# Earlier tanh, later read-state copy and other moves in the hand-written order of an attention and two-MoE kernel

## The chip, the cores and the metric

The kernel runs on one NeuronCore of one Trainium2 chip. The metric is the device time of one execution in microseconds (us). TensorE (PE in the profile) multiplies matrices, ScalarE (ACT) computes activation functions, VectorE (DVE) does elementwise work and reductions, GpSimd (POOL) issues the scatters, SyncE (SP) issues most of the loads. The engines run on their own and meet through semaphores; each of them takes its own instructions in the order of the program.

## What is computed

```python
scores = scale * x @ state.T            # per batch (4) and head (8): 512 tokens, 32 states, 64 wide
a = softmax(scores);   xread = a @ state
a2 = softmax(scale * state @ x.T);  sread = a2 @ x
x = concat([xread, sread], axis=2)      # -> 2304 rows of 512
h = x @ w_in                            # 512 -> 2048
g = h * tanh(softplus(h))               # mish
x = g @ w_out                           # 2048 -> 512
# then: normalise, 8 logits per row, argmax expert, out = gate * relu(x @ w1[e]) @ w2[e]
```

All is float32. A product of two float32 matrices is made of three products of a rounded part (hi) and a remainder (lo): hi·hi, lo·hi and hi·lo.

## The kernel before

**Stages.** The first 400 us or so are attention and the first MoE; the rest is a loop over tiles of 128 rows, one after the other, each through its expert. The change touches the first stage alone. There the rows come in four chunks c = 0 to 3 of 512 tokens, one for each batch, and a fifth, z, of 128 rows, the read state `sread` of all batches. The 2048 hidden columns of a chunk are 8 pairs p = 0 to 7 of 256 columns; z has two units of 512 columns, z0 and z1. `SEQ` lists these 34 units in the order in which ACT and DVE work on them: pair v = 8c + p is unit u = v up to v = 26, then come z0 (u = 27), pair 27 (28), z1 (29) and the pairs 28 to 31 (30 to 33).

**Weights.** `xread @ w_in` is computed as attention weights times M, with M = state @ w_in: four blocks M(c, nb) for each chunk. PE makes a block from w_in (L535), ACT writes its hi part (`M_hi`, L957), DVE its lo part (`M_lo`, L1341).

**One unit u of mish** goes through these steps, each of them one instruction over 128 x 1024 numbers:

- PE: `H(v)`, the hidden pair, 12 matmuls into two PSUM banks (L597); HB for z (L622).
- ACT: `mish_t` t, tanh (L1026); `mish_w` w, a square (L1030); `mish_b`, b, two exponentials (L1036, L1038), a seed for a reciprocal; `mish_c` c, a square (L1042); `mish_hi` hi (L1049).
- DVE: `mish_q` q (L1479), after w, which reads the PSUM banks of H for the last time; `mish_e` e (L1484), after b; `mish_r` r (L1489); `mish_g` g (L1496), after c and r; `mish_lo` lo (L1502), after hi.
- PE: `Y(v)`, the product with w_out, 24 matmuls (L641), after lo. A chunk's output gathers in four PSUM banks over its 8 pairs.

**Order.** Each engine's order is written out by hand. PE in iteration v: `H(v + 2)`, side work, `Y(v)`, side work. H(v + 2) waits for q of unit v + 1, since it writes into the banks that q reads. DVE in iteration u: q(u), lo(u - 1), side work, e(u), r(u), side work, g(u), side work. ACT in iteration u before the change: t(u), w(u), hi(u - 1), side work, b(u), side work, c(u), side work, and then t(u + 1).

**Side work**, laid into the iterations by pair number:

- attention of the next chunk: `score` (PE, L506, waits for M_lo of the last block of the present chunk, whose PSUM bank it takes), `scores_out` (ACT, L968), `soft_1` (DVE, L1387 to L1391, after scores_out and behind g of pair 2), `exp_1` (ACT), `soft_3`, `soft_4`, `soft_2` and `soft_5` (DVE), `exp_2` (ACT), `A_hi` and `A_lo` (L986, L1431), `turn_x` (DVE, L1362), `sread` (PE, L551), `sread_scale` (DVE, L1440), `sread_turned` (PE, L562) and `sread_out` (ACT, L994 and L997), the copy of the read state.
- output and routing of the chunk before, called `done`: `y_out` (ACT L1065 and DVE L1520), for which the next chunk's first Y waits, since it writes the same banks; `squares` (ACT, L1078); `route_t` (PE, L684), a transpose of one tile of 128 rows; `turned` (ACT, L1086), its copy out of PSUM; `route_l` (PE, L705), the logits from that copy; `parts_out` (ACT, L1091); `route_s` (PE, L712), after parts_out; `route_k`; `route_a` and `route_b` (DVE, L1528 to L1549 and L1557 to L1574), whose last step is the index by which POOL scatters the chunk.

In chunk 3, PE's iteration v = 28 begins H(30), route_l(2, 3), the first half of Y(28), route_s(2). route_l(2, 3) waits for `turned(2, 3)`, which ACT has in iteration u = 31 behind c(31), before and after the change.

The functions that the change touches, with the lines that the profile names:

Of the kernel before, what the change touches and what calls it, by code (L numbers as in the profile page):

```python
# [41 lines left out]
def build(nc, x, state, w_in, w_out, emb, tau, w1, w2, out):  # L42
# [70 lines left out]
    with ExitStack() as ctx:  # L113
# [383 lines left out]
        def _(pe):  # L497
# [297 lines left out]
            for v in range(B * PC):  # L795
# [28 lines left out]
                if c == 3:  # L824
                    if p == 2:
                        route_t(2, 0)
                    if p == 3:
                        route_l(2, 1)
                        route_t(2, 2)
                    if p == 4:  # L830
                        route_l(2, 3)
                        Y(v, (0,))
                        route_s(2)
                    if p == 5:
                        route_k(2)
                    if p == 6:
                        YB(0)
                    if p == 7:
                        Y(v, (0,))
                        TY(t0)  # L840
                Y(v, (1,) if v == 0 or c in (1, 2) and p == 3 or c == 3 and p in (4, 7) else (0, 1))
                if v < 2:
# [8 lines left out]
                if c == 0:  # L851
                    if p == 3:
                        score(1)
                    if p == 4:
                        sread_turned(0)
# [84 lines left out]
        def _(act):  # L940
# [218 lines left out]
            for u in range(1, PC):  # L1159
                mish_b(u)  # L1160
                if u == 6:
                    o_split(6)
                if u < PC - 1:
                    mish_t(u + 1)
# [3 lines left out]
                if u == PC - 1:  # L1168
                    o_split(7)
                    break  # L1170
                mish_w(u + 1)
                if u == 6:
                    A_hi(1)
# [10 lines left out]
                if u == 4:  # L1184
                    scores_out(1)
                    o_split(5)
                if u == 5:
                    exp_1(1)
                    sread_out(0)
            for u in range(PC, len(SEQ)):  # L1190
                kind, c, p = SEQ[u]
                n = p if kind == "m" else -1
                done = c - 1 if kind == "m" else -1
                mish_t(u)
                if n == (6 if c == 3 else 5):
# [6 lines left out]
                if done >= 0:  # L1202
# [4 lines left out]
                    if n == 5 and c == 3:  # L1207
                        turned(done, 2)
                if kind == "m" and (n in (0, 2) and c == 1 or n == 2 and c > 1):
                    M_hi(c, n + 1)  # L1210
# [6 lines left out]
                if n == 6 and c in (1, 2):  # L1217
                    A_hi(c + 1)
                mish_b(u)
                if (kind, p) == ("z", 1):  # L1220
                    turned(2, 0)
# [6 lines left out]
                if n == 2 and c in (1, 2):  # L1228
                    scores_out(c + 1)
                if done >= 0 and n == 1:  # L1230
                    y_out(done)
                    if c > 1:
                        M_hi(c, 2)
                mish_c(u)
                if c == 1 and n == 0:
                    M_hi(1, 2)
                if done >= 0:
                    if n == 2:
                        squares(done, (0, 1) if c < 3 else range(ST))
                    if n == 3 and c < 3:  # L1240
                        turned(done, 1)
                        squares(done, (2, 3))
                    if n == 4 and c < 3:
                        turned(done, 3)
                    if n == 5:
                        if c == 3:
                            turned(done, 3)
                        else:
                            gate_exp(done)
                    if n == 6 and c == 3:  # L1250
                        gate_exp(done)
                        split_gz(0)
                    if n == 7 and c == 3:
                        split_gz(1)
                if c in (1, 2):
                    if n == 4:
# [78 lines left out]
        def _(dve):  # L1335
# [335 lines left out]
            for u in range(1, PC):  # L1671
                mish_e(u)
                mish_r(u)
                if u == 5:
                    sread_scale(0)
                if u == 6:
# [6 lines left out]
                if u == 6:  # L1683
                    A_lo(1)
                mish_lo(u)
                if u > 1:
                    o_rest(u)
# [16 lines left out]
            for u in range(PC, len(SEQ)):  # L1704
                kind, c, p = SEQ[u]
                n = p if kind == "m" else -1
                done = c - 1 if kind == "m" else -1
                if done >= 0 and n == (7 if c == 3 else 6):
                    route_b(done)
                mish_q(u)  # L1710
                if SEQ[u - 1][0] == "m":
                    mish_lo(u - 1)
                if done >= 0 and n == (6 if c == 3 else 5):
                    route_a(done)
                if n == 7 and c in (1, 2):
                    M_lo(c + 1, 1)
                if kind == "m" and (n in (0, 2) and c == 1 or n == 2 and c > 1):
                    M_lo(c, n + 1)
# [4 lines left out]
                if n == 4 and c in (1, 2):  # L1723
                    soft_2(c + 1)
                mish_e(u)
                mish_r(u)
                if n == 6 and c in (1, 2):
                    M_lo(c + 1, 0)
                if n == 1 and c > 1:
                    M_lo(c, 2)  # L1730
                if done >= 0 and n == 1:
                    y_out(done)
                mish_g(u)
                if n == 0 and c > 1:
                    sread_scale(c)
                if c == 1 and n == 0:
                    M_lo(1, 2)
                if c in (1, 2):
                    if n == 0:
# [11 lines left out]
                if kind == "m" and c < 3:  # L1751
                    if n == 5 and c == 1:
                        sread_scale(1)
                    if n == 5 and c > 0:
                        soft_5(c + 1)
                    if n == 6 and c > 0:
                        A_lo(c + 1)
                if c == 3 and n == 6:
# [170 lines left out]
```

## Time and profile before

| | us |
|---|---|
| median of three runs | 672.82 |
| lowest and highest | 672.47, 672.86 |
| profiled execution | 672.58 |
| its span, first to last instruction | 670.8 |
| PE busy in the span | 644.4 |
| DVE busy | 442.9 |
| ACT busy | 387.4 |

The profiled execution lies between the lowest and the highest run; 1.8 us of it lie around the span. The clock granted to TensorE was 0.996 of full speed over the span. Read the table by engine first: the one that is nearly always busy sets the pace, and what is left to win is the time in which it sits idle and whom it waits for.

### The profile page before, as it was taken

The page shows a single profiled execution, that of the slowest core. Times are in us where ns is not written, and L with a number is a line of the kernel's source. Part 1 is how long each engine was busy: PE and PEld are TensorE (multiplying, and loading weights), DVE is VectorE, ACT ScalarE, POOL GpSimd, SP SyncE. Part 2 cuts the span into 40 slices and gives each one's busy share as a digit, 9 for nine tenths or more (in the row PEclk, how much of TensorE's full clock was granted, in tenths as well). Part 3 has the DMA queues.
Part 4 walks back from the last instruction along what each step waited for, and adds up shares of the span by engine and source line. Part 5 has one row for each costly group of instructions (what it writes and reads, how often), then busy time and mean ns, then how long its engine had stood idle before and what let it go on. Part 6 is the DMA issues. An engine that isn't in the chain of part 4 may idle for free.

```text
span 670.8 us, 12454 instructions
## 1 busy us (share of the span) xinstructions
PE 644.4 (96%) x4174; PEld 496.0 (74%) x4175; DVE 442.9 (66%) x701; ACT 387.4 (58%) x501; POOL 51.0 (8%) x76
## 2 busy tenths in 40 slices
PE   7889999999999999999999999999999999999996
PEld 5666767577776777766678888788888888888884
DVE  6899899978688789775677677654512542272271
ACT  2789678687588685777787473444422531261260
POOL 2000000000200001100000213010000100100101
PEclk8999999999999999999999999999999999999999
DMA  8802546200433000515000632662711441063140
GB/s 256 246 33 95 191 131 199 78 2 2 128 127 95 32 2 33 158 52 192 9 1 1 250 96 97 235 237 88 241 32 38 166 161 47 32 208 136 41 163 6
DMA packets 35352, 72.73 MB, mean 108 GB/s; under 512 B 5700, under 2 KB 5700, under 8 KB 35313
## 3 DMA queue, kind: packets, MB, share of 16 engines
q1 hardware_dynamic: 27728, 56.93, 26.2%
q0 software_dynamic: 3040, 9.13, 3.5%
q10 hardware_dynamic: 4544, 6.14, 3.0%
q8 instruction: 26, 0.43, 0.3%
q14 instruction: 14, 0.11, 0.0%
HBM read 60.92 MB, written 12.16 MB: 109 GB/s over the span
## 4 chain that ended last, share of the span: by engine, by line
PE 65%; DVE 16%; ACT 9%; issue 5%; DMA 3%; ACTq 0%; SPq 0%; POOL 0%; DVEq 0%; POOLq 0%
PE PS L748 16%; PE PS L777 16%; PE PS L641 14%; PE PS L597 5%; DVE ww L1484 3%; PE PS L757 2%; PE PS L506 2%; PE PS L622 2%; ACT ww L1042 2%; DVE qq L1496 2%; ACT rr L1038 2%; DVE qq L1479 2%; PE PS L662 1%; ACT rr L1036 1%; PE PS L535 1%
## 5 line engine op out<-in xcount | busy, mean ns | idle before, releaser
L641 PE MATMUL PS<-WH,gh 128*128 128x512 f32 x256 | 103.9, 406 | 2.1 <-DVE ysb L1520 1.3
L641 PE MATMUL PS<-WH,gl 128*128 128x512 f32 x256 | 101.0, 395 | 0.0
L641 PE MATMUL PS<-WL,gh 128*128 128x512 f32 x256 | 100.9, 394 | 0.0
L1142 ACT ACTIVATE hh<-PS 128x512 fp32r<-128x512 f32 x40 | 21.9, 595 | 91.3 <-PE PS L757 88.2
L1578 DVE TENSOR_TENSOR WL<-raw,WH 128x1024 f32 (+1 forms) x48 | 56.0, 1220 | 19.2 <-ACT WH L1122 18.6
L777 PE MATMUL PS<-WH,hh 128*128 (+1 forms) x160 | 65.3, 408 | 0.0
L777 PE MATMUL PS<-WH,hl 128*128 (+1 forms) x160 | 63.0, 394 | 0.0
L777 PE MATMUL PS<-WL,hh 128*128 (+1 forms) x160 | 62.8, 393 | 0.0
L641 PEld LDWEIGHTS PS<-WH,gh 128*128 128x128 f32 x256 | 48.2, 188 | 19.3 <-issue 8.2
L1597 DVE TENSOR_SCALAR osb<-PS,gid 128x512 f32<-128x512 f32 x21 | 15.7, 749 | 66.8 <-PE PS L777 66.8
L1122 ACT ACTIVATE WH<-raw 128x1024 f32 (+1 forms) x48 | 47.6, 1054 | 20.1 <-issue 7.5
L1042 ACT ACTIVATE ww<-ww,cst 128x1024 f32<-128x1024 f32 (+1 forms) x35 | 39.4, 1126 | 34.1 <-DVE ww L1484 34.1
L641 PEld LDWEIGHTS PS<-WH,gl 128*128 128x128 f32 x256 | 48.2, 188 | 11.3
L1479 DVE SCALAR_TENSOR_TENSOR qq<-ww,PS 128x1024 f32<-128x1024 f32 (+1 forms) x35 | 41.4, 1183 | 22.4 <-ACT ww L1030 22.4
L641 PEld LDWEIGHTS PS<-WL,gh 128*128 128x128 f32 x256 | 48.3, 189 | 10.0
L1134 ACT ACTIVATE hsb<-PS 128x512 f32<-128x512 f32 x42 | 24.3, 593 | 51.8 <-PE PS L748 44.1
L1484 DVE SCALAR_TENSOR_TENSOR ww<-ww,rr 128x1024 f32<-128x1024 f32 (+1 forms) x35 | 41.6, 1188 | 17.8 <-ACT rr L1038 17.7
L748 PE MATMUL PS<-WH,yh 128*128 (+1 forms) x168 | 47.7, 405 | 1.5 <-DVE yl L1583 1.5
L597 PE MATMUL PS<-Ah,WH 128*128 128x512 f32 x124 | 42.7, 425 | 6.1 <-DVE qq L1479 5.1
L1583 DVE TENSOR_TENSOR yl<-PS,yh 128x512 fp32r<-128x512 f32 x21 | 14.4, 688 | 48.2 <-ACT yh L1128 48.2
L1496 DVE SCALAR_TENSOR_TENSOR qq<-ww,qq 128x1024 f32<-128x1024 f32 (+1 forms) x33 | 39.3, 1190 | 10.2 <-ACT ww L1042 10.2
L748 PE MATMUL PS<-WH,yl 128*128 (+1 forms) x168 | 46.0, 395 | 0.0
(275 smaller groups left out, 1245.6 us busy)
## 6 DMA issues: line engine op xcount, KB each, us to landing
raw<-in_w SPq DMA_DIRECT2D x48, 512.0 KB, 3.3
raw<-in_w_in SPq DMA_DIRECT2D x36, 512.0 KB, 4.8
yg<-by_expert ACTq DMA_DIRECT2D x22, 260.0 KB
raw<-in_w_out SPq DMA_DIRECT2D x8, 512.0 KB, 5.0
by_expert<-junk SPq DMA_DIRECT2D x1, 2080.0 KB, 10.1
wr<-in_w_in SPq DMA_DIRECT2D x4, 512.0 KB, 9.1
x_0a<-in_x SPq DMA_DIRECT2D x8, 128.0 KB, 4.3
x_0b<-in_x SPq DMA_DIRECT2D x8, 128.0 KB, 4.8
```

The costliest lines, as they stand in the source:

```text
L597: mm = pe.matmul(PS[:, h_bank(v) + e, :], w[:, (NB * c + p // 2) % NM, o:o + P], a[:, c % 2, g, :], start=(i == 0 and g == 0), stop=(i == ...
L641: mm = pe.matmul(PS[:, 2 + t, :], a[:, v % 2, e, t * P:t * P + P], w[:, 8 + p, e * 512:e * 512 + 512], start=(p == 0 and e == 0 and i == 0 ...
L748: mm = pe.matmul(PS[:, j, :], a[:, k, :], w[:, bass.ds(slot + k, 1), j * 512:j * 512 + 512].rearrange("p o n -> p (o n)"), start=(i == 0 a ...
L777: mm = pe.matmul(PS[:, o_bank(t, end), :], a[:, m, :], w[:, bass.ds(slot + (KT + m // 2), 1), (m % 2) * 512:(m % 2) * 512 + 512].rearrange ...
L1042: a.activation(ww[:, u % 2, es], ww[:, u % 2, es], ACT.Square, bias=cst[:, 0:1]).then_inc(s_rdy, 1)
L1122: a.activation(WH[:, bass.ds(slot + b, 1), :].rearrange("p o n -> p (o n)"), raw[:, b % NSTAGE], ACT.Copy).then_inc(w_hi, 1)
L1134: a.activation(hsb[:, j * 512:j * 512 + 512], PS[:, j, :], ACT.Relu).then_inc(hs_rdy, 1)
L1142: a.activation(hidden(end)[0][:, 4 * j:4 * j + 4, :], PS[:, 3 + j, :].rearrange("p (k m) -> p k m", k=4), ACT.Copy).then_inc(hh_rdy, 1)
L1479: v.scalar_tensor_tensor(out=qq[:, u % 2, es], in0=ww[:, u % 2, es], scalar=4.0, in1=PS[:, bank + es.start:bank + es.stop, :], op0=ALU.sub ...
L1484: v.scalar_tensor_tensor(out=ww[:, u % 2, es], in0=ww[:, u % 2, es], scalar=4.0, in1=rr[:, es], op0=ALU.add, op1=ALU.mult).then_inc(e_rdy, 1)
L1496: v.scalar_tensor_tensor(out=to, in0=ww[:, u % 2, es], scalar=0.75, in1=qq[:, u % 2, es], op0=ALU.add, op1=ALU.mult).then_inc(g_rdy, 1)
L1578: v.tensor_tensor(WL[:, bass.ds(slot + b, 1), :].rearrange("p o n -> p (o n)"), raw[:, b % NSTAGE], WH[:, bass.ds(slot + b, 1), :].rearran ...
```

## The change

No instruction is added or taken away. Moved are:

- ACT, units 8 to 33: tanh of the next unit, t(u + 1), stands ahead of c(u) where the next unit is a pair, at the end of the iteration where it is z. (Up to unit 7 it stood ahead of c already.)
- ACT: `turned(done, 1)` and `turned(done, 3)` of chunks 0 and 1 go ahead of that t and of c; `sread_out(0)` from the end of unit 5 to behind b(6); `exp_1(1)` ahead of hi(5); `y_out(0)` ahead of b(9); `M_hi(1, 3)` from unit 10 to behind b(9).
- DVE: `sread_scale(0)` behind lo(5), `sread_scale(2)` and `(3)` ahead of g; `y_out(0)` ahead of e(9); `M_lo(1, 3)` from unit 10 to behind g(9); `route_b` of chunks 0 and 1 from ahead of q to behind lo; `A_lo(2)` and `A_lo(3)` from behind g to behind that route_b, ahead of e.
- PE: the first half of Y(3) stands behind H(5), `score(1)` between the halves; the first half of Y(26) ahead of route_t(2, 0).

```diff
--- before.py
+++ after.py
@@ -823,6 +823,7 @@
                     M(c + 1, p - 5)
                 if c == 3:
                     if p == 2:
+                        Y(v, (0,))
                         route_t(2, 0)
                     if p == 3:
                         route_l(2, 1)
@@ -838,7 +839,10 @@
                     if p == 7:
                         Y(v, (0,))
                         TY(t0)
-                Y(v, (1,) if v == 0 or c in (1, 2) and p == 3 or c == 3 and p in (4, 7) else (0, 1))
+                if v == 3:
+                    Y(v, (0,))
+                    score(1)
+                Y(v, (1,) if v in (0, 3) or c in (1, 2) and p == 3 or c == 3 and p in (2, 4, 7) else (0, 1))
                 if v < 2:
                     M(0, v + 2)
                 if c in (1, 2):
@@ -849,8 +853,6 @@
                         route_l(c - 1, 2)
                         route_t(c - 1, 3)
                 if c == 0:
-                    if p == 3:
-                        score(1)
                     if p == 4:
                         sread_turned(0)
                 if c < 3:
@@ -1160,6 +1162,7 @@
                 mish_b(u)
                 if u == 6:
                     o_split(6)
+                    sread_out(0)
                 if u < PC - 1:
                     mish_t(u + 1)
                 if u == 6:
@@ -1169,6 +1172,8 @@
                     o_split(7)
                     break
                 mish_w(u + 1)
+                if u == 5:
+                    exp_1(1)
                 if u == 6:
                     A_hi(1)
                 mish_hi(u)
@@ -1184,14 +1189,11 @@
                 if u == 4:
                     scores_out(1)
                     o_split(5)
-                if u == 5:
-                    exp_1(1)
-                    sread_out(0)
+            mish_t(PC)
             for u in range(PC, len(SEQ)):
                 kind, c, p = SEQ[u]
                 n = p if kind == "m" else -1
                 done = c - 1 if kind == "m" else -1
-                mish_t(u)
                 if n == (6 if c == 3 else 5):
                     parts_out(done)
                 mish_w(u)
@@ -1206,7 +1208,7 @@
                         turned(done, 2)
                     if n == 5 and c == 3:
                         turned(done, 2)
-                if kind == "m" and (n in (0, 2) and c == 1 or n == 2 and c > 1):
+                if kind == "m" and (n == 0 and c == 1 or n == 2 and c > 1):
                     M_hi(c, n + 1)
                 if c > 1 and n == 1:
                     sread_out(c)
@@ -1216,7 +1218,13 @@
                     exp_1(c + 1)
                 if n == 6 and c in (1, 2):
                     A_hi(c + 1)
+                if c == 1 and n == 1:
+                    y_out(done)
                 mish_b(u)
+                if c == 1 and n == 1:
+                    M_hi(1, 3)
+                if n in (3, 4) and 0 < c < 3:
+                    turned(done, (1, 3)[n - 3])
                 if (kind, p) == ("z", 1):
                     turned(2, 0)
                 if c == 3 and n == 4:
@@ -1227,10 +1235,11 @@
                     M_hi(c + 1, 0)
                 if n == 2 and c in (1, 2):
                     scores_out(c + 1)
-                if done >= 0 and n == 1:
+                if c > 1 and n == 1:
                     y_out(done)
-                    if c > 1:
-                        M_hi(c, 2)
+                    M_hi(c, 2)
+                if u < LAST and SEQ[u + 1][0] == "m":
+                    mish_t(u + 1)
                 mish_c(u)
                 if c == 1 and n == 0:
                     M_hi(1, 2)
@@ -1238,10 +1247,7 @@
                     if n == 2:
                         squares(done, (0, 1) if c < 3 else range(ST))
                     if n == 3 and c < 3:
-                        turned(done, 1)
                         squares(done, (2, 3))
-                    if n == 4 and c < 3:
-                        turned(done, 3)
                     if n == 5:
                         if c == 3:
                             turned(done, 3)
@@ -1252,6 +1258,8 @@
                         split_gz(0)
                     if n == 7 and c == 3:
                         split_gz(1)
+                if u < LAST and SEQ[u + 1][0] == "z":
+                    mish_t(u + 1)
                 if c in (1, 2):
                     if n == 4:
                         exp_2(c + 1)
@@ -1671,8 +1679,6 @@
             for u in range(1, PC):
                 mish_e(u)
                 mish_r(u)
-                if u == 5:
-                    sread_scale(0)
                 if u == 6:
                     M_lo(1, 0)
                 mish_g(u)
@@ -1683,6 +1689,8 @@
                 if u == 6:
                     A_lo(1)
                 mish_lo(u)
+                if u == 5:
+                    sread_scale(0)
                 if u > 1:
                     o_rest(u)
                 if u == 1:
@@ -1705,16 +1713,19 @@
                 kind, c, p = SEQ[u]
                 n = p if kind == "m" else -1
                 done = c - 1 if kind == "m" else -1
-                if done >= 0 and n == (7 if c == 3 else 6):
+                if c == 3 and n == 7:
                     route_b(done)
                 mish_q(u)
                 if SEQ[u - 1][0] == "m":
                     mish_lo(u - 1)
+                if c in (1, 2) and n == 6:
+                    route_b(done)
+                    A_lo(c + 1)
                 if done >= 0 and n == (6 if c == 3 else 5):
                     route_a(done)
                 if n == 7 and c in (1, 2):
                     M_lo(c + 1, 1)
-                if kind == "m" and (n in (0, 2) and c == 1 or n == 2 and c > 1):
+                if kind == "m" and (n == 0 and c == 1 or n == 2 and c > 1):
                     M_lo(c, n + 1)
                 if c == 1 and n == 0:
                     soft_2(1)
@@ -1722,19 +1733,23 @@
                     soft_5(1)
                 if n == 4 and c in (1, 2):
                     soft_2(c + 1)
+                if c == 1 and n == 1:
+                    y_out(done)
                 mish_e(u)
                 mish_r(u)
                 if n == 6 and c in (1, 2):
                     M_lo(c + 1, 0)
                 if n == 1 and c > 1:
                     M_lo(c, 2)
-                if done >= 0 and n == 1:
+                if c > 1 and n == 1:
                     y_out(done)
-                mish_g(u)
                 if n == 0 and c > 1:
                     sread_scale(c)
+                mish_g(u)
                 if c == 1 and n == 0:
                     M_lo(1, 2)
+                if c == 1 and n == 1:
+                    M_lo(1, 3)
                 if c in (1, 2):
                     if n == 0:
                         turn_x(c + 1, 0)
@@ -1753,8 +1768,6 @@
                         sread_scale(1)
                     if n == 5 and c > 0:
                         soft_5(c + 1)
-                    if n == 6 and c > 0:
-                        A_lo(c + 1)
                 if c == 3 and n == 6:
                     lo_gz(0)
                 if c == 3 and n == 7:
```

## Rows read from the trace of the kernel before

**Rows 1.** Busy time, share of the span and instructions of each engine, from the page.

```profile
PE 644.4 (96%) x4174; PEld 496.0 (74%) x4175; DVE 442.9 (66%) x701; ACT 387.4 (58%) x501; POOL 51.0 (8%) x76
```

**Rows 2.** Timeline of PE, 98 to 335 us: start, duration, instruction [idle before <-releaser].

```profile
99.85 0.71 PE L597 MATMUL PS<-Ah,WH 128*128 128x512 f32 x2 [0.94 <-issue]
...
124.47 0.48 PE L641 MATMUL PS<-WH,gh 128*128 128x512 f32 x1 [1.30 <-DVE ysb L1520]
...
147.40 0.43 PE L705 MATMUL PS<-yTr,enT 128*32 128x128 f32 x8 [1.00 <-ACT yTr L1086]
...
189.03 0.72 PE L597 MATMUL PS<-Ah,WH 128*128 128x512 f32 x2 [0.39 <-DVE qq L1479]
...
237.34 0.43 PE L705 MATMUL PS<-yTr,enT 128*32 128x128 f32 x8 [1.02 <-ACT yTr L1086]
...
264.94 0.74 PE L597 MATMUL PS<-Ah,WH 128*128 128x512 f32 x2 [1.42 <-DVE qq L1479]
...
290.82 0.41 PE L562 MATMUL PS<-ident,shn 128*64 128x128 f32 x2 [0.52 <-DVE shn L1440]
...
333.32 0.63 PE L684 MATMUL PS<-ident,ysb 128*128 128x128 f32 x4 [0.92 <-DVE qq L1479]
```

**Rows 3.** Waits of ACT: engine, line, released by: us in total, times, longest.

```profile
ACT ww L1042 <- DVE ww L1484: 34.1, 27, 2.5
...
ACT ww L1026 <- PE PS L597: 7.9, 7, 1.7
```

**Rows 4.** Timeline of DVE at 98 us: A_lo(1), for which H(8) waits.

```profile
98.53 1.22 DVE L1431 TENSOR_TENSOR Al<-AF,Ah 128x1024 fp32r<-128x1024 f32 x1
```

**Rows 5.** Timeline of PE: end of H(11), route_l(0, 0) behind Y(9), start of H(12).

```profile
136.08 0.62 PE L597 MATMUL PS<-Ah,WL 128*128 128x512 f32 x2
...
142.64 0.43 PE L705 MATMUL PS<-yTr,enT 128*32 128x128 f32 x8
...
143.41 0.71 PE L597 MATMUL PS<-Ah,WH 128*128 128x512 f32 x2
```

**Rows 6.** Timeline of ACT, 134 to 138 us: scores_out(2), c(10), t(11).

```profile
134.01 1.02 ACT L968 ACTIVATE SC<-PS 128x1024 f32<-128x1024 f32 x1 [4.43 <-PE PS L506]
134.94 1.14 ACT L1042 ACTIVATE ww<-ww,cst 128x1024 f32<-128x1024 f32 x1
...
137.35 1.01 ACT L1026 ACTIVATE ww<-PS 128x1024 f32<-128x1024 f32 x1
```

**Rows 7.** Timeline of DVE, 136 to 142 us: g(10), soft_1(2) (first and last of three), q(11).

```profile
136.18 1.22 DVE L1496 SCALAR_TENSOR_TENSOR qq<-ww,qq 128x1024 f32<-128x1024 f32 x1 [2.37 <-ACT ww L1042]
137.32 1.24 DVE L1387 STREAM_TRANSPOSE PT<-SC 128x1024 f32<-128x1024 f32 x1
...
139.92 1.23 DVE L1391 TENSOR_TENSOR PT<-PT,r 128x1024 f32<-128x1024 f32 x1
141.06 1.21 DVE L1479 SCALAR_TENSOR_TENSOR qq<-ww,PS 128x1024 f32<-128x1024 f32 x1
```

**Rows 8.** Timeline of DVE at 219 us: M_lo(2, 3).

```profile
218.88 1.21 DVE L1341 TENSOR_TENSOR WL<-PS,WH 128x1024 fp32r<-128x1024 f32 x1
```

**Rows 9.** Timeline of DVE, 261 to 264 us: route_b(1), first and last of 14.

```profile
261.60 0.15 DVE L1557 TENSOR_REDUCE small<-lg 128x4 f32<-128x32 f32 x1
...
263.59 0.17 DVE L1574 CAST idx<-small 128x4 uint32<-128x4 f32 x1
```

**Rows 10.** Timeline of PE: last matmuls of H(30), then route_l(2, 3).

```profile
353.23 0.61 PE L597 MATMUL PS<-Ah,WL 128*128 128x512 f32 x2
353.77 0.42 PE L705 MATMUL PS<-yTr,enT 128*32 128x128 f32 x8
```

**Rows 11.** Timeline of ACT, 350 to 355 us: c(31), turned(2, 3), t(32).

```profile
350.91 1.15 ACT L1042 ACTIVATE ww<-ww,cst 128x1024 f32<-128x1024 f32 x1 [1.29 <-DVE ww L1484]
351.96 0.58 ACT L1086 ACTIVATE yTr<-PS 128x512 f32<-128x512 f32 x1
353.88 1.03 ACT L1026 ACTIVATE ww<-PS 128x1024 f32<-128x1024 f32 x1 [1.34 <-PE PS L597]
```

## The prediction, made before the changed kernel was run

> **What bounds the kernel now.** I read the page's busy times first. PE is busy for 644.4 of 670.8 us and its clock is 0.996 of full speed, so the time is PE's work plus the places where PE stands still [rows 1]. No instruction is added or dropped, so the change can only move PE's idle time, 26.4 us in the whole span. Next I went through PE's timeline for all of its waits between 98 us, where the change begins to act, and 400 us, where the tile loop takes over. There are eight of more than 0.2 us, 0.94 + 1.30 + 1.00 + 0.39 + 1.02 + 1.42 + 0.52 + 0.92 = 7.5 us [rows 2]. That is all that the change can win. Then the waits of ACT: in front of c it idles 27 times, 34.1 us in all, 1.26 us each, since e on DVE ends that much after b. In front of t it waits for H only 7 times [rows 3]. The change puts t into the first of these holes. What the reader is to see is why the second figure is small: t today comes when H is long done.
>
> **The parts that aim at a wait.** Each is followed by order alone, with the durations of the rows.
>
> - Chunk 0. With score(1) half a Y earlier, scores_out(1) and soft_1(1) start earlier and two holes of DVE close (1.2 and 0.5 us). sread_scale and sread_out leave the way of g(5) and of b(6). A_lo(1) ends at about 98.9 instead of 99.75 us [rows 4], and the wait of H(8), 0.94 us (the page says issue, but it ends 0.1 us after A_lo), nearly goes. PE's order itself costs nothing: score(1) needs an M_lo that is done by then.
> - y_out(0) ahead of e(9) and b(9). Y(8) no longer waits for the copy: 1.30 us gone. M(1, 3)'s split moves with it, so score(2) finds its bank free.
> - turned(., 1) ahead of t: the two waits of 1.00 and 1.02 us at route_l go.
> - route_b behind q and lo: 14 small instructions, from 261.60 to 263.67, 2.1 us [rows 9], leave the way of q(14) and q(22); the waits 0.39 and 1.42 us are theirs.
> - sread_scale(3) ahead of g: 0.52 us. First half of Y(26) ahead of route_t(2, 0), which waits for q of z1: 0.92 us, covered by 2.9 us of matmuls.
>
> Taken alone these would give the full 7.5 us.
>
> **Tanh ahead of c.** This part has a price. ACT works in order. t(u + 1) needs H(u + 1). If ACT reaches it before H(u + 1) has ended, ACT stops, and c(u), whose input is ready, stops behind it; so do g(u), the side work behind g on DVE, and then q(u + 1), for which the next H waits. I compared, unit by unit, the start of c(u) with the end of H(u + 1). H ends after c starts in 16 of the 24 units from 8 to 32 whose successor is a pair, by 0.6 to 2.9 us. Add the 0.95 us of t itself and c(u) comes later by 1.5 to 3.9 us in these. Where the side work is small that is free: from the end of H(u + 1) it takes t 0.95, c 1.15, g 1.35, q 1.25 = 4.7 us to q, and PE has Y(u - 1) for 5.7 us meanwhile. Where it isn't, PE waits:
>
> - Unit 10. Today: scores_out(2) ends at 135.0, c(10) follows at once at 134.94, t(11) only at 137.35 [rows 6]; g(10) at 136.18, soft_1(2) from 137.32, q(11) at 141.06 to 142.27 [rows 7]. PE reaches H(12) at 143.41, 1.1 us after q [rows 5]. H(11) ends at 136.7. After the change PE is 1.8 us earlier, so H(11) ends at 134.9; then t to 135.95, c 135.85 to 137.0, g 137.15, soft_1 138.3 to 142.1, q to 143.25, H(12) at 143.35. Work could go on at 141.65, so 1.7 us are waited, and all that was won up to here is gone.
> - The same for H(10) (c(8) is held by t(9), turn_x behind g(8)): 0.45 us; H(13): 0.5; route_s(0), since parts_out comes behind exp_2 behind c(12) behind t(13): 0.7. With 0.05 left at H(8) the new waits up to H(16) are 3.4 us against 3.63 today: PE is 0.2 to 0.3 us earlier there.
> - Chunk 2 has no early y_out as chunk 1 does. c(16) waits for H(17) and starts 3.6 us later; hi(16) and b(17) follow. So M_lo(2, 2) is late for M(2, 3), 1.0 us, y_out(1) [rows 8] for Y(16), 0.2, and M_lo(2, 3), which today ends as score(3) starts [rows 8], 0.35. Then unit 18 repeats unit 10: 1.8 at H(20); 0.5 at H(21), 0.8 at route_s(1). At H(23) route_b is out of the way, but q(22) stands behind soft_5(3), which is late with g(21): 1.0. M(3, 0) waits 0.15 for the index of the later route_b. Before chunk 3, M(3, 3) and Y(24) as before: 1.0 and 0.2. Sum 7.0 against 1.02 + 1.42 + 0.52 = 2.96 today: PE is 3.7 us late at Y(24).
> - Chunk 3. z0 and z1 keep t at the end, and in z0 the hole helps. turned(2, 0) waits for the later route_t(2, 0), t(30), c(29) and q(30) come after it: 1.2 us more at H(29). Then a wait that cannot be filled. In PE's order H(30) is followed directly by route_l(2, 3) [rows 10], which needs turned(2, 3), which ACT has behind c(31) [rows 11], and c(31) now stands behind t(32), which needs H(30). So PE stands from the end of H(30) for t 0.95 + c 1.05 + turned 0.6 plus hand-over, 2.8 us, wherever the engines are at that point. Today turned(2, 3) is over at 352.54, 1.2 us ahead.
> - The end of the stage. ACT and DVE arrive about 9.7 us late at first_expert and the scatter, PE 6.7 us. The slack in front of y_out(3) takes up most of it: 1.4 us more at route_t(3, 0). Sum of chunk 3: 5.4 against 0.92.
>
> **A rule beside it.** The Trainium skill, page "PSUM — Partial Sum Buffer", section "Engine vs sequencer instructions", says that the queues of ScalarE and VectorE are strictly first in, first out. It speaks against this change: nothing overtakes a tanh that waits. By it the losses stand as worked out; if c could pass, the 15.8 us of new waits would shrink to the few tenths left at H(8), and the time would be near 665. No row of the trace before can show it directly, since wherever t waits there, nothing behind it is ready.
>
> **Sum.** New waits 3.4 + 7.0 + 5.4 = 15.8, less 7.5 (and 0.1 that I lose in rounding): +8.2 us. The profiled execution took 672.58, the median of the runs is 672.82; I set the sum on the first: 680.8 us. Busy time doesn't change, and the tile loop from 430 us on only shifts.
>
> **Rivals.**
>
> 1. *All waits go.* t ahead of c costs nothing, since c's dependents have slack: 7.5 us won, 665.1. For it: up to unit 7 the order is already so and PE waits little there. Against: 2.8 us at route_l(2, 3) don't depend on slack. It decides at q(u + 1): as long as it ends 5.7 us after H(u + 1). 5%.
> 2. *Balance.* The side work overlaps better than I count, the new waits of chunks 1 and 2 are half of mine (5.2) and chunk 3 adds the forced 2.8: about the time before, 671 to 674. 10%.
> 3. *Slower, but by less.* Chunk 1 wins its 1.8 us to some part and chunk 2 loses half (3.5): 674.5 to 678. 23%.
> 4. *Slower by more.* The late first_expert makes the first expert's weights late as well. wlo of block 3 ends 10.5 us ahead of the first expert matmul today, so 3 us of extra delay are covered, but the scatter of z and the third tile hang on the same chain: up to 4 us more, 683 to 687. 12%.
>
> The forecast itself, 678 to 683: 50%. The range 674.3 to 685.0 leaves out rival 1, most of rival 2 and the end of rival 4. A measurement of this kernel can tell about 0.2%, 1.3 us, from no change. Faster by more than that: 8%; within: 7%; slower: 85%.
>
> **What the profile after would show.** Right: ACT's waits in front of t for H rise from 7 times 1.1 us to some 16, with more than 25 us in all, and those in front of c shrink; PE waits 2.8 us at route_l(2, 3), released by the copy yTr of ACT, and more than 1 us each at H(12) and H(20), released by q; Y(8) and the two route_l of tile 1 wait no more. Wrong: if PE's order gave H(u + 1) earlier than I read, t would find it done, and c would start at once. The forecast also falls if the parts that aim at a wait leave more slack on DVE than the 1.1 us at H(12) and H(20).

## The result and the profile after

The changed kernel takes 681.76 us (median; 680.5 to 682.99), the kernel before 672.84 (672.47 to 674.2). The ratio is 1.0132, with a 95% interval of 1.0108 to 1.0156: 8.9 us slower. The forecast was 680.8. The profiled execution took 680.5 us, with a span of 678.7; before it was 672.58 and 670.8. The instructions are the same, but PE is busy for 647.1 instead of 644.4 us; its granted clock is 0.993 over the span, before it was 0.996. So of the 7.9 us by which the spans differ, 5.2 are idle time of PE and 2.7 are busy time.

First the span in five stretches that end at the same PE instruction in both kernels: the starts of H(8), H(16), Y(24) and the second expert tile, and the end. The columns are the stretch, its length and the busy time of each engine with the number of its instructions, the granted clock, and DMA. After:

```profile
0.00:98.49 98.49, 88.54 (x685) 66.72 (x686) 87.01 (x119) 70.32 (x86) 4.51 (x28) 0.98 0.53 158
98.49:187.80 89.31, 86.62 (x694) 63.06 (x695) 76.40 (x106) 65.43 (x83) 6.96 (x8) 1.00 0.28 86
187.80:304.38 116.58, 110.45 (x1060) 80.51 (x1053) 90.03 (x118) 84.03 (x98) 6.12 (x5) 1.00 0.21 69
304.38:420.41 116.03, 110.69 (x543) 83.15 (x543) 77.17 (x155) 74.42 (x97) 14.42 (x14) 0.99 0.25 87
420.41:678.70 258.29, 250.79 (x1203) 205.42 (x1201) 111.51 (x207) 91.77 (x139) 20.58 (x22) 1.00 0.35 121
```

The same stretches of the kernel before:

```profile
0.00:99.85 99.85, 88.25 (x685) 65.40 (x686) 87.14 (x119) 69.84 (x86) 4.34 (x28) 0.98 0.51 158
99.85:189.03 89.18, 86.46 (x695) 62.89 (x695) 75.79 (x106) 66.16 (x84) 5.61 (x8) 1.00 0.29 91
189.03:301.73 112.70, 109.63 (x1053) 80.27 (x1053) 90.89 (x118) 84.19 (x97) 6.01 (x5) 1.00 0.20 64
301.73:411.97 110.24, 108.96 (x550) 82.21 (x543) 77.50 (x155) 75.33 (x98) 14.46 (x14) 1.00 0.27 94
411.97:670.80 258.83, 251.06 (x1203) 205.21 (x1201) 111.61 (x207) 91.88 (x139) 20.59 (x22) 1.00 0.35 121
```

The differences are -1.4, +0.1, +3.9, +5.8 and -0.5 us, 7.9 in all. Chunk 0 wins, chunk 1 comes out even, chunks 2 and 3 lose.

Three of the waits of PE in the changed kernel, from its timeline, at H(10), H(12) and route_l(2, 3):

```profile
119.24 0.73 PE L597 MATMUL PS<-Ah,WH 128*128 128x512 f32 x2 [0.38 <-DVE qq L1487]
...
142.38 0.73 PE L597 MATMUL PS<-Ah,WH 128*128 128x512 f32 x2 [1.40 <-DVE qq L1487]
...
359.25 0.66 PE L705 MATMUL PS<-yTr,enT 128*32 128x128 f32 x8 [2.63 <-ACT yTr L1088]
```

and the largest totals of those that matter here, over the whole span (the first holds 2.36 us at 43 us, ahead of everything that the change moves):

```profile
PE PS L597 <- DVE qq L1487: 8.2, 8, 2.4
PE PS L705 <- ACT yTr L1088: 2.6, 1, 2.6
PE PS L535 <- DVE WL L1349: 2.1, 2, 1.1
PE PS L712 <- ACT junk L1093: 1.4, 2, 0.7
PE PS L684 <- DVE ysb L1528: 1.1, 1, 1.1
```

None of the eight waits of [rows 2] is left with its size and cause: H(23) waits 0.86 instead of 1.42 us. New are 0.38 at H(10), 1.40 at H(12), 0.69 at route_s(0), 1.05 at M(2, 3), 1.40 at H(20), 0.69 at route_s(1), 0.41 at M(3, 0), 1.05 at M(3, 3), 1.38 at H(29), 2.63 at route_l(2, 3) and 1.15 at route_t(3, 0). With H(23) and four small ones that is 13.9 us against 7.7 before, where the 7.5 us of [rows 2] leave out one of 0.17 us at H(29).

The waits of ACT, which answer to [rows 3], name the cause:

```profile
ACT ww L1028 <- PE PS L597: 41.4, 19, 6.4
...
ACT ww L1044 <- DVE ww L1492: 12.6, 14, 2.9
```

Tanh now waits for H 19 times, for 41.4 us, where it waited 7 times and 7.9 us, and c for e for 12.6 where it waited 34.1. The hole in front of c is filled, but more by waiting than by work.

The longest new wait, at H(30). ACT after, which answers to [rows 11]: t(32), c(31), turned(2, 3):

```profile
356.65 1.02 ACT L1028 ACTIVATE ww<-PS 128x1024 f32<-128x1024 f32 x1 [3.09 <-PE PS L597]
357.57 1.14 ACT L1044 ACTIVATE ww<-ww,cst 128x1024 f32<-128x1024 f32 x1
358.61 0.59 ACT L1088 ACTIVATE yTr<-PS 128x512 f32<-128x512 f32 x1
```

H(30) ends at 356.6, the copy at 359.20, and PE goes on at 359.25. The input of c(31) had long been there, as the row of e(31) on DVE shows; it ended at 354.81:

```profile
353.59 1.22 DVE L1492 SCALAR_TENSOR_TENSOR ww<-ww,rr 128x1024 f32<-128x1024 f32 x1 [1.39 <-ACT rr L1040]
```

So c(31) stood behind t(32) for 2.8 us with all that it needs. Behind PE's wait the second to sixth matmul of Y(28) start 0.43 us apart instead of 0.23. The granted clock (third column from the end) shows why, in a stretch up to the end of the wait and one behind it:

```profile
354.00:359.00 5.00, 2.62 (x12) 1.83 (x10) 2.14 (x3) 2.35 (x3) 0.00 (x0) 0.99 0.00 0
359.20:361.00 1.80, 1.75 (x11) 1.18 (x12) 0.84 (x1) 1.03 (x2) 0.00 (x0) 0.50 0.02 5
```

The clock stood at 1.2 instead of 2.4 GHz there, and this half of Y took 4.2 us instead of 3.05: 1.1 us more that no wait shows.

### The profile page after: what moved, and what is told of

It reads as the page before. It is cut to its first block, busy times and chain, and to the rows that moved or that the text cites. A ratio compares the mean times of both kernels' runs of the same rounds, so it can differ in the third digit from the quotient of the medians.

```text
span 678.7 us, 12455 instructions
## 1 busy us (share of the span) xinstructions
PE 647.1 (95%) x4174; PEld 498.9 (74%) x4175; DVE 442.1 (65%) x701; ACT 386.0 (57%) x501; POOL 52.6 (8%) x76
## 4 chain that ended last, share of the span: by engine, by line
PE 68%; DVE 15%; ACT 7%; issue 4%; DMA 3%; SPq 0%; ACTq 0%; POOL 0%; DVEq 0%; POOLq 0%
PE PS L748 16%; PE PS L777 16%; PE PS L641 14%; PE PS L597 10%; ACT ww L1044 2%; PE PS L757 2%; DVE qq L1504 2%; PE PS L622 2%; PE PS L551 2%; DMA raw<-in_w 2%; DVE qq L1487 2%; PE PS L506 2%; ACT ww L1028 1%; PE PS L729 1%; DVE ww L1492 1%
## 5 line engine op out<-in xcount | busy, mean ns | idle before, releaser
L1028 ACT ACTIVATE ww<-PS 128x1024 f32<-128x1024 f32 (+1 forms) x35 | 34.8, 995 | 46.1 <-PE PS L597 41.4
L1605 DVE TENSOR_SCALAR osb<-PS,gid 128x512 f32<-128x512 f32 x21 | 15.7, 749 | 67.0 <-PE PS L777 67.0
L641 PEld LDWEIGHTS PS<-WH,gl 128*128 128x128 f32 x256 | 48.7, 190 | 11.5
L1044 ACT ACTIVATE ww<-ww,cst 128x1024 f32<-128x1024 f32 (+1 forms) x35 | 39.3, 1122 | 12.6 <-DVE ww L1492 12.6
```

Of the source, the lines that this page charges most:

```text
L641: mm = pe.matmul(PS[:, 2 + t, :], a[:, v % 2, e, t * P:t * P + P], w[:, 8 + p, e * 512:e * 512 + 512], start=(p == 0 and e == 0 and i == 0 ...
L1028: a.activation(ww[:, u % 2, es], PS[:, bank + es.start:bank + es.stop, :], ACT.Tanh, scale=0.5).then_inc(t_rdy, 1)
L1044: a.activation(ww[:, u % 2, es], ww[:, u % 2, es], ACT.Square, bias=cst[:, 0:1]).then_inc(s_rdy, 1)
```

## The experiments

Two theories stand against each other. **The queue theory**: ACT stops in a tanh whose H isn't done, and what is behind it comes late. **The rival**: the other moves, a later route_b with the scatter, y_out ahead of e and b, cost as well or instead.

**e1. Tanh back, all other moves kept.** The last two lines stand at the end of each unit. (In this and the following diffs `...` marks what is left out.)

```diff
-                if u < LAST and SEQ[u + 1][0] == "m":
-                    mish_t(u + 1)
                 mish_c(u)
...
-                if u < LAST and SEQ[u + 1][0] == "z":
-                    mish_t(u + 1)
...
+                if u < LAST:
+                    mish_t(u + 1)
```

> The changed kernel with tanh of the next unit put back behind c and the side work, all other moves kept. Queue theory (ScalarE stops in tanh, c and all behind it come late): the new waits of 15 us go and seven of the eight old ones stay away, so some 7 us below the kernel before: 665 to 667 us; PE waits only tenths at H(12), H(20) and route_l(2, 3). Rival (the other moves cost as well, the later route_b with the scatter, and y_out in front of e and b): 670 us or more. Rival (tanh ahead of c helps in part, and only route_l(2, 3) costs): about 673.

Measured: 666.59 us (666.04 to 667.0), ratio to the kernel before 0.9902 (0.9882 to 0.9922). PE's waits between 98 us and the tile loop are 0.36 at route_s(0), 0.41 at M(3, 0) and this one at H(29):

```profile
334.29 0.73 PE L597 MATMUL PS<-Ah,WH 128*128 128x512 f32 x2 [1.27 <-DVE qq L1485]
```

So the other moves together win 6.4 us, and the order of the tanh, which is all in which this kernel differs from the changed one, costs 15.2 us.

**e2. The tanh order alone.** The kernel before with t(u + 1) ahead of c(u), nothing else.

> The kernel before with nothing changed but tanh ahead of c in units 8 to 32. Queue theory: slower than the changed kernel, since the copies turned(., 1) and turned(., 3) of chunks 0 and 1 now stand behind t and c as well, and PE has route_l directly behind the H that t waits for: four more waits of 2.6 us like that at route_l(2, 3), partly instead of others. 688 to 694 us. Rival (the slow-down comes from the other moves): at or below 673 us.

Measured: 714.05 us (713.15 to 717.07), ratio 1.062 (1.0588 to 1.0653). The direction is the queue theory's, the size is not: 41 us instead of 15 to 21. The waits of PE:

```profile
PE PS L705 <- ACT yTr L1086: 13.2, 5, 2.6
PE PS L597 <- DVE qq L1483: 10.9, 8, 2.9
PE PS L562 <- DVE shn L1444: 7.7, 2, 3.9
```

The five times 2.64 us at route_l were expected: each has its copy behind c and itself directly behind the H for which t waits. I had overlooked `sread_turned(2)` and `(3)`. They too stand directly behind an H, and need `sread_scale`, which in this kernel comes behind g behind c. ACT and DVE at the first of them:

```profile
215.15 1.02 ACT L1026 ACTIVATE ww<-PS 128x1024 f32<-128x1024 f32 x1 [4.90 <-PE PS L597]
216.07 1.14 ACT L1042 ACTIVATE ww<-ww,cst 128x1024 f32<-128x1024 f32 x1
...
217.31 1.23 DVE L1500 SCALAR_TENSOR_TENSOR qq<-ww,qq 128x1024 f32<-128x1024 f32 x1 [4.67 <-ACT ww L1042]
218.46 0.47 DVE L1444 TENSOR_SCALAR shn<-PS,r 128x64 f32<-128x64 f32 x2
```

t, c, g and the scale in a row are 3.87 us of standing PE, twice. I had also counted the clock nowhere: PE's busy time is 655.9 us instead of 644.4 for the same matmuls. The waits between 98 us and the tile loop are 36.0 us, 28.5 more than before; with the 11.5 us of busy time that is 40.0 of the 40.6 us by which the spans differ. The clock stood at half in five stretches, two of them shown at the end of this text. This also tells what the moves of `turned(., 1)`, `turned(., 3)` and `sread_scale(2)`, `(3)` are in the change: they repair most of what the early tanh breaks. Without the early tanh all the other moves are worth 6.4 us, with it 32.3.

**e3. Tanh ahead of c only where it is free.** Of the 23 units, the seven in which H of the next unit ended before c could start.

```diff
+            AHEAD = (8, 14, 15, 22, 23, 27, 29)
...
-                if u < LAST and SEQ[u + 1][0] == "m":
+                if u in AHEAD:
                     mish_t(u + 1)
                 mish_c(u)
...
+                if u < LAST and u not in AHEAD:
+                    mish_t(u + 1)
```

> The changed kernel with tanh ahead of c only in the seven units in which H of the next unit ends before c could start (8, 14, 15, 22, 23, 27, 29). Queue theory: no new waits, as e1, 665 to 667 us, equal to e1 within 1 us because the holes of ScalarE that it fills are on no chain that PE waits for by now. If tanh in the hole of c is worth something where it is free, it is 1 to 2 us below e1.

Measured: 666.26 us (666.18 to 669.82), ratio 0.9913 (0.9879 to 0.9946), the same as e1. PE waits 0.41 at H(10), 0.25 at route_s(0), 0.37 at M(3, 0) and 1.38 at H(29). Filling the hole of c is worth nothing there. In unit 8 it costs: ACT has no hole in front of c(8), since exp_2(1) fills it, so t(9), whose H is done, only puts itself ahead of a c(8) that could go.

```profile
112.72 1.01 ACT L1028 ACTIVATE ww<-PS 128x1024 f32<-128x1024 f32 x1
113.63 1.14 ACT L1044 ACTIVATE ww<-ww,cst 128x1024 f32<-128x1024 f32 x1
```

These are t(9) and c(8) of e3; e(8) had ended at 112.39. In e1 there is no wait at H(10). The prediction had this term, 0.45 us; calling unit 8 free for e3 left out that ACT must also be idle there.

**e4. The one copy that was left behind.** The changed kernel with turned(2, 3) ahead of t(32).

```diff
+                if c == 3 and n == 5:
+                    turned(2, 3)
                 if u < LAST and SEQ[u + 1][0] == "m":
                     mish_t(u + 1)
...
-                    if n == 5:
-                        if c == 3:
-                            turned(done, 3)
-                        else:
-                            gate_exp(done)
+                    if n == 5 and c < 3:
+                        gate_exp(done)
```

> The changed kernel with one more move: turned(2, 3) of unit 31 ahead of t(32), as chunks 0 and 1 have it. Queue theory: the wait of 2.6 us at route_l(2, 3) goes, and with it the stretch at half clock that followed it (1.1 us), the rest stays: 3 to 4 us below the changed kernel, 677.5 to 679 us. Rival (the lateness of chunk 3 comes from elsewhere and only shows there): less than 1.5 us.

Measured: 678.59 us (678.35 to 680.5), ratio to the kernel before 1.0086 (1.006 to 1.0112): 3.2 us below the changed kernel. The wait at route_l(2, 3) is gone; all the others stand as they were, to 0.05 us, but the one at route_t(3, 0), 0.49 instead of 1.15, with a new one of 1.21 at TY(0) for its DMA. The sum fits: 2.63 and 1.1 of clock and 0.66 less, 1.21 more, are 3.2 us. The price of one misplaced instruction of 0.6 us is thus about 3 us.

**e5. One late c in the kernel before.** t(32) ahead of c(31), nothing else.

```diff
-                mish_t(u)
...
+                if u == 31:
+                    mish_t(u + 1)
                 mish_c(u)
...
+                if u < LAST and not (u == 31):
+                    mish_t(u + 1)
```

> The kernel before with tanh ahead of c in one place only, t(32) ahead of c(31). Queue theory: PE, which does not wait there now, waits 2.6 us at route_l(2, 3) and runs the next half of Y at half clock (1.1 us more, if the clock falls after such a wait as in the changed kernel): 676 to 677 us with the clock, 675.3 without. Rival (one late c is absorbed by slack): within 1 us of the kernel before.

Measured: 677.27 us (676.03 to 678.56) against 672.93, ratio 1.0058 (1.0038 to 1.0078). PE's timeline shows the one wait added, and the clock behind it:

```profile
357.49 0.43 PE L705 MATMUL PS<-yTr,enT 128*32 128x128 f32 x8 [2.64 <-ACT yTr L1086]
...
358.88 0.46 PE L641 MATMUL PS<-WL,gh 128*128 128x512 f32 x1
359.13 0.63 PE L641 MATMUL PS<-WH,gl 128*128 128x512 f32 x1
359.56 0.63 PE L641 MATMUL PS<-WH,gh 128*128 128x512 f32 x1
```

2.64 us of standing and matmuls at 0.43 us instead of 0.23. No slack took it up. The profiled execution, 677.65 us, has a second stretch at half clock, behind the wait at 44 us, which has nothing to do with the edit; the median is 0.3 us above what was expected.

**e6. The pattern of unit 10 alone.** The kernel before with t(11) ahead of c(10) and t(19) ahead of c(18), the two units in which soft_1 stands behind g.

> The kernel before with t(11) ahead of c(10) and t(19) ahead of c(18) only, the two units with soft_1 behind g. Queue theory: c starts 2.7 us later, H(12) and H(20) wait 1.7 us each, and the copies turned(., 1) behind b and c of the next unit come 2.8 us later, so that route_l(., 1) waits 2 us instead of 1: 2.8 us for each of the two chunks, 678.5 us. Rival (only the 1.7 us at H count): 676.2. Rival (slack of 1.1 us and more absorbs it): 673 to 674.

Measured: 678.91 us (678.26 to 680.17), ratio 1.0086 (1.0064 to 1.0107), 6.0 us for two moved instructions. H(12) and H(20) wait 1.40 us each, route_l(0, 1) and route_l(1, 1) 2.07 and 2.04 instead of 1.00 and 1.02: 2.5 us for each chunk. Behind the second of these two equal waits the clock fell, behind the first it did not (granted clock 1.00 and 0.64):

```profile
150.70:155.00 4.30, 4.30 (x28) 3.44 (x29) 4.13 (x6) 4.24 (x8) 1.05 (x1) 1.00 0.00 0
243.30:248.00 4.70, 4.70 (x23) 3.64 (x24) 4.53 (x6) 4.64 (x9) 1.04 (x1) 0.64 0.03 7
```

Y(18) took 1.5 us longer for it. The wait of 1.42 us at H(23) shrank to 0.33, as DVE had caught up by then. The sum was right, its make-up only in part.

**e7 and e8. Two of the winning moves alone.** e7 moves route_b(0), route_b(1), A_lo(2) and A_lo(3) on DVE, e8 moves y_out(0) and the split of M(1, 3) on ACT and DVE.

> The kernel before with only route_b of chunks 0 and 1 and A_lo(2), A_lo(3) moved on VectorE. The waits of 0.39 us at H(16) and 1.42 us at H(23) go, a few tenths may come at M(3, 0), which needs the index: 671.0 to 671.6 us. Rival (A_lo ahead of e delays e and gives it back): 672.5 or more.

Measured: 671.75 us (671.47 to 675.17) against 672.93, ratio 0.9995 (0.9972 to 1.0017). The trace has the mechanism: no wait at H(16) and H(23), one of 0.50 us new at sread_turned(2). The time, 1.2 us less in the medians, is within its uncertainty.

> The kernel before with only y_out(0) and the split of M(1, 3) moved. The wait of 1.30 us at Y(8) goes and score(2) starts by as much earlier; nothing takes it back where c(10) still follows scores_out(2) at once: 671.5 us. In the changed kernel this gain was lost at H(12), and by the queue theory because of t(11) alone. Rival (it is lost at H(12) here too, since soft_1 is the bound): 672.8.

Measured: 671.82 us (669.59 to 674.33), ratio 0.998 (0.9959 to 1.0001). No wait at Y(8) and none at H(12); 0.3 us come back at route_l(0, 1), which waits 1.28. So the gain at Y(8) is lost at H(12) in the changed kernel by t(11), not by soft_1. As a time the gain can't be told from none.

**e10. The moves in chunk 0 alone**: half of Y(3), exp_1(1), sread_out(0), sread_scale(0).

> The kernel before with the moves in chunk 0 only: half of Y(3) ahead of score(1), exp_1(1) ahead of hi(5), sread_out(0) behind b(6), sread_scale(0) behind lo(5). A_lo(1) comes 0.9 us earlier and the wait of 0.94 us at H(8) goes: 671.9 us. Rival (the wait marked as issue is one of instruction supply): 672.8.

Measured: 672.53 us (670.78 to 674.33) against 673.58, ratio 0.9975 (0.9954 to 0.9995). The wait at H(8) is gone; the gain of 1.1 us is only just clear of noise. The stop marked issue in sread(0), 1.01 us before, is 1.78 us here and 0.99 to 1.40 in the other runs. In the kernel before and in e2, e5, e6, e7 and e8, which have the same order up to there, it is 1.01 to 1.23, so part of it moves from execution to execution; whether the order adds to it isn't shown.

**e9, e11 and e12c. What holds H(29).** In e1 PE still waits 1.27 us there. I took it for the copy turned(2, 0), which waits for a route_t that the change put half a Y later. e9 puts that copy behind c(29):

```diff
-                if (kind, p) == ("z", 1):
-                    turned(2, 0)
...
                 mish_c(u)
+                if (kind, p) == ("z", 1):
+                    turned(2, 0)
```

> e1 (tanh back behind c, all other moves) with one more: turned(2, 0) of unit 29 behind c(29) instead of ahead of it. In e1 PE waits 1.27 us at H(29), since turned(2, 0) waits for the later route_t(2, 0) and c(29) waits behind it. Queue theory: c(29) goes on, the wait at H(29) goes, route_l(2, 0) still finds its copy: 1.2 us below e1, 665.4 us. Rival (the bound there is the DVE or H(28) itself): as e1.

Measured: 667.38 us (667.06 to 669.06), and the wait grew:

```profile
336.34 0.73 PE L597 MATMUL PS<-Ah,WH 128*128 128x512 f32 x2 [1.76 <-DVE qq L1485]
```

This theory fell. ACT of e1 shows why: the copy lay in the hole in front of c and held nothing up, as c(29) waits for e(29), which ends at 329.79; behind c it holds up t(30) by the 0.5 us that PE waits longer.

```profile
329.31 0.60 ACT L1088 ACTIVATE yTr<-PS 128x512 f32<-128x512 f32 x1 [0.78 <-PE PS L684]
329.82 1.16 ACT L1044 ACTIVATE ww<-ww,cst 128x1024 f32<-128x1024 f32 x1
330.88 1.01 ACT L1028 ACTIVATE ww<-PS 128x1024 f32<-128x1024 f32 x1
```

e11 puts the first half of Y(26) back behind route_t(2, 0) in e1:

> e1 with the first half of Y(26) back behind route_t(2, 0). PE then waits 0.92 us at route_t(2, 0) as before the change, and the 1.27 us at H(29) shrink to about 0.2: within 0.3 us of e1, 666.6. By the forecast of the single parts (0.92 us won) it would be 0.9 us slower, 667.5.

Measured: 666.66 us (666.34 to 668.51), as e1. The waits are 0.92 at route_t(2, 0), 0.17 at H(29) and 0.36 at route_t(3, 0), 1.45 in all against 1.27. So the move of Y(26) wins nothing: it carries the wait from one place to the next.

e12c is e3, in which t(30) stands in the hole, with turned(2, 0) behind w(30).

```diff
+                    if n == 4 and c == 3:
+                        turned(2, 0)
...
-                if (kind, p) == ("z", 1):
-                    turned(2, 0)
```

> e3 (tanh ahead of c in the seven units where H is done by then) with turned(2, 0) in unit 30 behind w(30), so that between b(29) and w(30) ScalarE has only t(30), in the hole of c, and c(29). In e9 PE waited for t, w and q of unit 30 behind e(29) and c(29), not for the copy. Queue theory: t(30) runs 0.9 us before c(29) can start, w(30) follows c(29) at once, q(30) comes 1 us earlier and the wait at H(29) falls from 1.4 to 0.3 us: 665.3 us, 1 us below e3. Rival (route_l(2, 0) now waits for its copy): as e3, 666.3.

Measured: 666.46 us (665.12 to 668.87), ratio 0.9912 (0.9879 to 0.9946). H(29) waits no more, and of the 1.38 us this is left at route_l(2, 0). The waits are what the queue theory expects, but for this one of the rival; the time, expected at 665.3 by the one and at 666.3 by the other, doesn't show the gain:

```profile
332.42 0.43 PE L705 MATMUL PS<-yTr,enT 128*32 128x128 f32 x8 [0.41 <-ACT yTr L1088]
```

Its profiled execution is the shortest of all, 665.12 us, but the medians of e1, e3, e11 and e12c, 666.3 to 666.7, can't be told apart. Each of the four beats both kernels, by 6 to 7 us and by 15 us.

## Why the prediction was right, point by point

**The bound.** Right in the main, but that busy time doesn't change was wrong. PE's busy time grew by 2.7 us, and its idle time by 5.2 where the forecast has 8.2. The three middle stretches, 9.8 us longer together (forecast 8.9), have 7.1 us more idle and 2.7 us more busy time. Of these, 1.1 us are the half clock behind route_l(2, 3). The remaining 1.6 us are, by an estimate, waiting as well: a wait is counted from the modelled end of the last matmul before it, 0.24 us later than the next one could have started at H(12), and the changed kernel has eight more waits there.

**The parts that aim at a wait.** Right in mechanism, one by one, and in their sum: e1 is 6.4 us faster where the eight waits were 7.5. One was mis-sized: the 0.92 us at route_t(2, 0). e11 shows that it is worth nothing, since H(29) waits next; the sum of the single parts should have been 6.6. I had this chain in the part on chunk 3, but put it down to the early tanh. e1, without the early tanh, has the 1.27 us at H(29) all the same.

**Tanh ahead of c.** Right, and shown by e1, e2, e5 and e6: the order of the tanh alone is the 15.2 us between e1 and the changed kernel, where my sum has 15.7 (665.1 to 680.8). The signs in the profile came as forecast: 19 waits of tanh for H with 41.4 us (some 16 and more than 25 were forecast), 2.63 us at route_l(2, 3), 1.40 at H(12) and H(20), none at Y(8) and at the two route_l of tile 1. The count of units is 16 of 23, not of 24. The stretches up to H(8), H(16), Y(24) and the second expert tile should have gone by -0.9, +0.6, +3.9 and +4.4; they went by -1.4, +0.1, +3.9 and +5.8. The single terms, forecast and measured:

| place | forecast | measured |
|---|---|---|
| up to H(16): H(10), H(12), H(13), route_s(0) | 0.45, 1.7, 0.5, 0.7 | 0.38, 1.40, 0.22, 0.69 |
| M(2, 3), Y(16) | 1.0, 0.2 | 1.05, 0.20 |
| score(3) | 0.35 | under 0.2 |
| H(20), H(21), route_s(1) | 1.8, 0.5, 0.8 | 1.40, 0.22, 0.69 |
| H(23), M(3, 0) | 1.0, 0.15 | 0.86, 0.41 |
| M(3, 3), Y(24) | 1.0, 0.2 | 1.05, 0.20 |
| H(29) above 0.17, route_l(2, 3), route_t(3, 0) | 1.2, 2.8, 1.4 | 1.2, 2.63, 1.15 |

The largest error in one place is 0.4 us, at H(20). Together the measured ones are 13.8 us, where the forecast has 15.8. The terms at H(10) to H(23) are all too large, by 0.1 to 0.4, mostly because they measure another thing: mine count from where the next H could have started, the profile from the modelled end of what stands before it. At H(12) the transposes start at 140.33 and H could follow 0.41 us later, as H(30) does at 353.63 behind those of 353.22; it started at 142.38, 1.64 us after that, forecast 1.7 and 1.40 by the profile.

**What I missed.** The clock behind route_l(2, 3), 1.1 us, which is most of what chunk 3 lost above the forecast. Against it stand 0.5 us less in each of the first two stretches and in the tile loop; so the profiled execution came out at 680.5, forecast 680.8. The closeness is in part luck of these signs. In the first stretch the wait at H(8) went as forecast, but the rest of the figure has nothing to do with the moves: the first half of Y(0) started 1.16 us earlier than in the kernel before, H lost 1.2 us to half clock at 45 us, and a wait of 0.74 us at 63 us didn't come. The median is 1 us above the forecast, inside the range. Small slips: that range leaves out all of the second rival (671 to 674) and not most of it, and route_b ends at 263.76, not 263.67 [rows 9].

**The rule beside it.** The rule of strict order that the Trainium skill gives in "PSUM — Partial Sum Buffer", section "Engine vs sequencer instructions", speaks against the change. The trace agrees: ACT stands still for 3.09 us in front of t(32), and c(31), whose input was there at 354.81, starts at 357.57, 0.92 us after t(32).

**The rivals.** All waits go (665.1): this is what e1 measures, 666.6, but with the tanh put back. Balance, and slower by less, fell with e5 and e6, where what had been added was not absorbed. Slower by more fell with the changed kernel itself: from the second expert tile on it took 258.3 us, before 258.8. In e4 TY(0) waits 1.21 us for its DMA, which is all that was seen of that chain.

## What to carry to other kernels

An instruction moved forward in an in-order queue to fill a hole takes along what it waits for: compare, unit by unit, when its input is there with when the instruction behind it could start, and move it only where the first comes earlier and the engine would be idle until then. Here the first held in 7 of 23 units; in one of them there was no hole and H(10) waited 0.4 us for it, and in all together it won nothing that shows in the time. What the busiest engine wants directly behind the instruction that the moved one waits for must not stand behind it, or every pass costs a fixed sum, here 2.6 us over one more queue and 3.9 over two. And a wait taken away is worth something only as far as the next wait on the same chain: undo each part on its own before it is counted.

## What the runs showed of the hardware

After waits of PE of about the same length the granted clock fell in some executions and in others not. The cleanest case stands at 44 us, ahead of everything that the change moves. All 14 profiles have a wait there, at the same H for the same q, of 2.32 to 2.37 us. With it the clock fell in four of them (the changed kernel, e4, e5 and e12c) and stayed at 1.00 in the other ten. The kernel before and the changed kernel:

```profile
46.00:48.50 2.50, 2.50 (x12) 2.07 (x11) 2.46 (x5) 2.47 (x4) 0.00 (x0) 1.00 0.01 3
45.00:47.50 2.50, 2.50 (x8) 1.93 (x7) 2.46 (x5) 2.22 (x3) 0.00 (x0) 0.50 0.01 3
```

H took 4.2 us in the second instead of 3.0. e6 has the same twice in one execution, with 2.07 and 2.04 us. Behind the 2.63 and 2.64 us at route_l(2, 3) of the changed kernel and of e5 it fell both times. e2 has eight waits of 2.6 us or more: the clock fell at three of the five of 2.64 us and at both of 3.87, not at the one of 2.94 and at the other two. Twice it stayed at half for nearly 7 us:

```profile
218.30:224.90 6.60, 5.92 (x15) 4.71 (x16) 6.55 (x11) 3.80 (x5) 0.00 (x0) 0.50 0.00 0
273.00:279.30 6.30, 6.00 (x22) 4.51 (x22) 5.08 (x7) 6.11 (x10) 0.00 (x0) 0.50 0.00 0
```

In e10 it fell behind the stop of 1.78 us at 84 us, the longest of its kind. So a wait of PE has two prices, its length and at times a stretch at half clock, which stands in the busy time: 1.1 us at route_l(2, 3), 1.5 at Y(18) of e6, and 2.4 at 273 us in e2, where a half of Y took 5.3 instead of 2.9 us. What decides whether the clock falls, these rows don't show.

The other thing is the start: the first half of Y(0) starts between 31.41 and 34.37 us in these profiles, before any of the changes acts. That alone makes differences of 1 us hard to tell in the times, while they are plain in the waits.
